# q, k and v laid out by chunk in DRAM, and no transposes of q and k, in a kernel of chunked attention and two mixtures of experts

## The chip, the cores and the metric

The kernel runs on one core of one Trainium2 chip. The core has five engines that run their own instruction streams and meet only through semaphores: TensorE (PE in the profile; its loads of the stationary operand are shown apart as PEld), VectorE (DVE), ScalarE (ACT), GpSimd (POOL) and SyncE (SP), which in this kernel only issues DMAs. Sixteen DMA engines move data between DRAM and the on-chip memory SBUF. The metric is the time of one execution on the device, in microseconds (us); lower is better.

## What is computed

Three stages follow each other. With 4 batches, 8 heads, 576 positions and 64 values per head there are 2304 tokens of 512 values.

```python
# attention inside chunks of 64 positions
q_c = q.reshape(B, H, nc, chunk, D)           # 4, 8, 9, 64, 64; k_c and v_c alike
scores = scale * np.matmul(q_c, k_c.transpose(0, 1, 2, 4, 3))
scores = scores - np.max(scores, axis=-1, keepdims=True)
attn = np.exp(scores)
attn = attn / (np.sum(attn, axis=-1, keepdims=True) + 1e-09)
out = np.matmul(attn, v_c)
x = np.ascontiguousarray(out.transpose(0, 2, 1, 3)).reshape(B * S, H * D)
# first mixture: all 4 experts, weighted
for e in range(4):
    h = np.maximum(x @ w1[e], 0.0)
    out += p[:, e:e + 1] * (h @ w2[e])
# second mixture: each token goes to the one of 8 experts with the largest logit
expert_idx = np.argmax(x @ w_gate, axis=1)
out[mask] = gate_w[mask, None] * (np.maximum(x[mask] @ w1[e], 0.0) @ w2[e])
```

All of it is float32. The inner size of the experts is 1024.

## The kernel before, in words

A tile is 128 tokens, that is two chunks of 64 positions with all 8 heads; there are 18 tiles, worked on in 6 groups of 3 (`TG`). Expert products are done with each operand split into a high and a low part, so a product is three matmuls; they are the lines 1214 to 1216 (first layer, `hidden`, 384 tokens wide) and 1245 to 1247 (second layer, `output`, 512 wide).

Attention of one tile has these stages. Its q and k come to `qin` and `kin` with tokens and heads on the partitions. PE transposes them (four transposes each, lines 1122 and 1127) into two PSUM banks; ACT copies q to `qT` in a block form whose other half is zero (`take_qT`, line 532), DVE copies k to `kT` (`take_kT`, line 709). PE multiplies them, one matmul for each head (`score`, line 1135). DVE subtracts the row maximum (`shift`, lines 715 and 716), ACT takes the exponential (line 537), DVE divides by the sum (`normalise`, lines 721 to 724). PE transposes the result (`transpose_p`, line 1143), ACT copies it (line 541), PE multiplies it with `vbd`, which holds v in block form (`attend`, line 1152), and ACT copies the result to `x` (line 549).

The attention of group 0 stands ahead of everything else ("the start" below). Its q and k arrive in staging tiles, `qst` and `kst`, and ACT and DVE first reorder them into `qin` and `kin` (lines 581 and 747). PE fills its pauses with matmuls on a tile of ones (`warm`, line 1182). Then come six groups for expert 0 of the first mixture; between their matmuls the attention of the *next* group is spread, by the table `STAGES`: a group has 16 steps (8 of `hidden`, 8 of `output`), and after a step PE, ACT and DVE each do the stages that the table names for it. So five groups (tiles 3 to 17) carry attention in this way. After them experts 1 to 3 and the second mixture run, which the change does not touch.

SP issues nearly all loads in one fixed order: the first q tiles, the first weight chunk, v of group 0 between further weight chunks, the small inputs, the rest of the 8 chunks of expert 0 (512 KB each), then q and k of tile 3 and of those behind. ACT issues the first k tiles. POOL rounds and splits each weight chunk of expert 0 (lines 442 and 436), and PE waits for chunk c before step 2c of the first group.

Of the kernel before, what the change touches and what calls it, by code (L numbers as in the profile page):

```python
# [5 lines left out]
def chunked_attention_then_two_moes(nc, q, k, v, domain_probs, w1, w2, w_gate, v1, v2, out):  # L6
# [10 lines left out]
    ds = bass.ds  # L17

    P = 128
    B, H, S, DH = q.shape  # L20
# [4 lines left out]
    C = 64  # L25
    NCH = S // C
    J = 4
    PJ = C // J
# [57 lines left out]
    qin = tile("qin", [P, TG, J, 2, DH], F32, a0)  # L86
    kin = tile("kin", [P, TG, J, 2, DH], F32, a0 + 6144)
    vbd = tile("vbd", [P, 2, KT, P], F32, a0 + 12288)
    qT = tile("qT", [P, H, P], F32, a0 + 16384)
    kT = tile("kT", [P, H, C], F32, a0 + 20480)  # L90
# [9 lines left out]
    qT0 = tile("qT0", [P, TG, H, P], F32, at["acc"] + 24576)  # L100
    kT0 = tile("kT0", [P, TG, H, C], F32, at["h"])
    qst = tile("qst", [P, TG, 2, J, DH], F32, at["h"] + 6144)
    kst = tile("kst", [P, TG, 2, J, DH], F32, at["h"] + 12288)
    assert at["acc"] + 36864 <= at["h"]
# [62 lines left out]
    def spare(name, shape, dtype):  # L167
# [3 lines left out]
        for n in shape[1:]:  # L171
# [24 lines left out]
    STAGES = {0: [("qk", 0)], 1: [("score", 0)], 4: [("p", 0), ("qk", 1)], 5: [("v", 0), ("score", 1)],  # L196
              8: [("p", 1), ("qk", 2)], 9: [("v", 1), ("score", 2)], 12: [("p", 2)], 13: [("v", 2)]}
# [9 lines left out]
    q_first = [sem(f"q_first{i}") for i in range(TG)]  # L207
    k_first = [sem(f"k_first{i}") for i in range(TG)]
# [44 lines left out]
    def chunk_of(src, g):  # L253

        a = src.rearrange("b h (n p j) d -> b n h p j d", n=NCH, j=J)
        return a[ds(g // NCH, 1), ds(g % NCH, 1)].rearrange("o u h p j d -> (o u h) p j d")

# [3 lines left out]
    with stack:  # L261
# [4 lines left out]
        def _(sp):  # L266
            def load_qk(t, j):

                for c in range(2):
                    for src, dst in ((q, qin), (k, kin)):  # L270
                        sp.dma_start(dst[:, j, :, c, :], chunk_of(src, t * 2 + c)).then_inc(qk_in[j], 16)

            def load_v(t, to=vbd[:, :, :, :], signal=v_in):

                for c in range(2):
                    g = t * 2 + c
                    for odd in range(2):
                        a = v.rearrange("b (r o) (n s) d -> b n o s r d", o=2, n=NCH)
                        a = a[ds(g // NCH, 1), ds(g % NCH, 1), odd].rearrange("o u s r d -> (o u s) r d")
                        sp.dma_start(to[odd * C:(odd + 1) * C, c, :, odd * DH:(odd + 1) * DH], a).then_inc(signal, 16)  # L280
# [33 lines left out]
            sp.wait_ge(sem("k_psum"), TG)  # L314
            load_qk(TG, 0)
            load_qk(TG + 1, 1)
            sp.wait_ge(sem("v_zeroed"), 1)
            load_v(TG)
            load_qk(TG + 2, 2)
# [84 lines left out]
        def _(pool):  # L404
# [6 lines left out]
            gp.memset(qT0[:, :, :, :], 0.0).then_inc(sem("q_zeroed"), 1)  # L411
            gp.memset(qT[:, :, :], 0.0).then_inc(sem("q_zeroed"), 1)
# [1083 lines left out]
```

## Time and profile before

| | |
|---|---|
| median of 3 runs | 1252.15 us (1249.66 to 1252.37) |
| the profiled execution, its own time | 1250.36 us |
| its span, from the first to the last instruction | 1248.6 us |
| PE busy | 1220.7 us of the span |
| TensorE clock granted, mean | 0.991 of full |
| DMA packets, bytes | 104449, 81.14 MB |
| packets under 512 B | 60831 |

Around the span lie 1250.36 - 1248.6 = 1.8 us that no instruction covers. A row of the timeline gives the start of a piece of work, how long it lasted and, in brackets, how long its engine had been idle and what ended that. Ends of matmuls are modelled, so the spacing of their starts tells what they cost.

### The profile page before, as it was taken

The numbers are of one execution on the slowest core, as the hardware profiler recorded it, in microseconds if no ns is written. First come the engines' busy times: TensorE is split into PE (matmuls) and PEld (weight loads), VectorE is DVE, ScalarE is ACT, GpSimd is POOL, SyncE is SP. The second block draws the span as 40 slices with busy tenths as digits, with TensorE's granted clock in tenths as the row PEclk, the third lists the DMA queues.
The fourth block names the chain that finished last, engine by engine and source line by source line (L and its number), as shares of the span: only waits on it lengthen the run. The fifth ranks groups of instructions, "written<-read, shape, count | busy, mean of one in ns | idle before, by whom it ended". The sixth has DMA issues, their size and how long they took to land.

```text
span 1248.6 us, 19074 instructions
## 1 busy us (share of the span) xinstructions
PE 1220.7 (98%) x6541; PEld 1082.1 (87%) x6542; DVE 475.4 (38%) x958; ACT 288.9 (23%) x455; POOL 316.9 (25%) x192
## 2 busy tenths in 40 slices
PE   8999999999999999999999999999997999999986
PEld 6999989989999999999999998899985888888875
DVE  5433434432222222222222223343355555555543
ACT  3322322323111113211111311222133011041420
POOL 7400000005000002300000601100047843085892
PEclk9999999999999999999999999999998999999998
DMA  7422122004000002100001300000174432272730
GB/s 203 117 51 50 37 59 51 21 9 135 1 0 0 0 0 84 50 0 0 0 0 35 100 26 27 0 25 25 63 189 121 122 122 94 65 241 79 245 131 21
DMA packets 104449, 81.14 MB, mean 65 GB/s; under 512 B 60831, under 2 KB 87071, under 8 KB 104418
## 3 DMA queue, kind: packets, MB, share of 16 engines
q1 hardware_dynamic: 99186, 68.67, 18.8%
q0 software_dynamic: 4416, 11.30, 2.8%
q10 hardware_dynamic: 816, 0.79, 0.2%
q8 instruction: 16, 0.26, 0.1%
q14 instruction: 15, 0.12, 0.0%
HBM read 71.12 MB, written 10.92 MB: 66 GB/s over the span
## 4 chain that ended last, share of the span: by engine, by line
PE 90%; SPq 3%; POOL 2%; DMA 1%; issue 1%; DVE 1%; ACT 1%; POOLq 0%; ACTq 0%; DVEq 0%
PE psum L1214 14%; PE psum L1216 14%; PE psum L1215 13%; PE psum L1245 10%; PE psum L1247 10%; PE psum L1246 10%; PE psum L1417 3%; PE psum L1419 3%; PE psum L1418 3%; PE psum L1135 2%; PE psum L1152 2%; POOL weights_r L436 2%; PE psum L1404 1%; PE psum L1264 1%; SPq L280 1%
## 5 line engine op out<-in xcount | busy, mean ns | idle before, releaser
L436 POOL TENSOR_TENSOR weights_r<-weights,weights_r 128x1024 fp32r<-128x1024 f32 x96 | 232.1, 2445 | 693.4 <-ACT weights_r L611 692.4
L1214 PE MATMUL psum<-xhi,weights_r 128*128 128x384 f32 x768 | 261.5, 340 | 1.1 <-DVEq L784 0.4
L1216 PE MATMUL psum<-xhi,weights_r 128*128 128x384 f32 x768 | 257.1, 335 | 0.0
L1215 PE MATMUL psum<-xlo,weights_r 128*128 128x384 f32 x768 | 256.9, 334 | 0.0
L1245 PE MATMUL psum<-weights_r,hhi 128*128 128x512 f32 x576 | 228.7, 397 | 0.0
L1247 PE MATMUL psum<-weights_r,hlo 128*128 128x512 f32 x576 | 225.1, 391 | 0.0
L1246 PE MATMUL psum<-weights_r,hhi 128*128 128x512 f32 x576 | 224.6, 390 | 0.0
L606 ACT ACTIVATE hhi<-psum 128x384 fp32r<-128x384 f32 x192 | 94.5, 492 | 507.9 <-PE psum L1216 507.4
L790 DVE SCALAR_TENSOR_TENSOR hlo<-psum,hhi 128x384 fp32r<-128x384 f32 x192 | 107.0, 557 | 264.1 <-ACT hhi L606 264.1
L611 ACT ACTIVATE weights_r<-weights 128x1024 fp32r<-128x1024 f32 x88 | 92.3, 1058 | 241.4 <-DMA weights<-in_moe_w 241.4
L1214 PEld LDWEIGHTS psum<-xhi,weights_r 128*128 128x128 f32 x768 | 144.3, 188 | 4.3 <-DVE xlo L738 2.1
L1215 PEld LDWEIGHTS psum<-xlo,weights_r 128*128 128x128 f32 x768 | 144.3, 188 | 0.7
L1216 PEld LDWEIGHTS psum<-xhi,weights_r 128*128 128x128 f32 x768 | 144.1, 188 | 0.0
L1247 PEld LDWEIGHTS psum<-weights_r,hlo 128*128 128x128 f32 x576 | 108.1, 188 | 23.3
L1246 PEld LDWEIGHTS psum<-weights_r,hhi 128*128 128x128 f32 x576 | 108.3, 188 | 20.8
L1245 PEld LDWEIGHTS psum<-weights_r,hhi 128*128 128x128 f32 x576 | 108.2, 188 | 20.4
L1417 PE MATMUL psum<-weights_r,hThi 128*128 (+1 forms) x184 | 74.8, 406 | 2.3 <-DVE hTlo L1039 2.3
L809 DVE SCALAR_TENSOR_TENSOR acc<-psum,dp,acc 128x512 f32 x36 | 25.2, 751 | 134.5 <-PE psum L1247 134.5
L1214 PE MATMUL psum<-weights_r,xThi 128*128 x176 | 71.0, 403 | 4.2 <-POOL weights_r L436 4.0
L1418 PE MATMUL psum<-weights_r,hThi 128*128 (+1 forms) x184 | 73.0, 397 | 0.0
L1419 PE MATMUL psum<-weights_r,hTlo 128*128 (+1 forms) x184 | 72.9, 396 | 0.0
L1216 PE MATMUL psum<-weights_r,xTlo 128*128 x176 | 69.0, 392 | 0.0
(178 smaller groups left out, 1216.3 us busy)
## 6 DMA issues: line engine op xcount, KB each, us to landing
weights<-in_moe_w SPq DMA_DIRECT2D x96, 512.0 KB, 5.6
vbd<-in_v SPq DMA_DIRECT2D x72, 64.0 KB, 2.4
x_rows<-xfin SPq DMA_DIRECT2D x18, 256.0 KB, 2.1
qin<-in_q SPq DMA_DIRECT2D x30, 128.0 KB
kin<-in_k SPq DMA_DIRECT2D x30, 128.0 KB
kst<-in_k ACTq DMA_DIRECT2D x6, 128.0 KB
qst<-in_q SPq DMA_DIRECT2D x6, 128.0 KB
meta<-slot_table SPq DMA_DIRECT2D x25, 1.0 KB, 3.1
```

The costliest lines, as they stand in the source:

```text
L436: gp.tensor_tensor(rounded(set_, 1, c), raw(set_, c), rounded(set_, 0, c).bitcast(F32), ALU.subtract).then_inc(sem("w_lo"), 1)
L606: sc.activation(hhi_r[:, f, :], psum[:, H_B[f], 0:G], ACT.Relu).then_inc(sem("hhi_ready"), 1)
L790: vec.scalar_tensor_tensor(hlo_r[:, f, :], psum[:, H_B[f], 0:G], 0.0, hhi[:, f, :], ALU.max, ALU.subtract).then_inc(sem("hlo_ready"), 1)
L1214: mm(out_, ahi, bhi, start=(i == 0), stop=False)
L1215: mm(out_, ahi, blo, start=False, stop=False)
L1216: last = mm(out_, alo, bhi, start=False, stop=(i == n - 1))
L1245: mm(o_, hhi_r[:, f, toks], mat2(W_r, 0, 0, f), start=(f == 0), stop=False)
L1246: mm(o_, hhi_r[:, f, toks], mat2(W_r, 1, 0, f), start=False, stop=False)
L1247: last = mm(o_, hlo_r[:, f, toks], mat2(W_r, 0, 0, f), start=False, stop=(f == FT - 1))
L1417: mm(psum[:, Y2_B, :], hThi_r[:, f, :], mat2(W_r, 0, off, f), start=(f == 0), stop=False)
L1418: mm(psum[:, Y2_B, :], hThi_r[:, f, :], mat2(W_r, 1, off, f), start=False, stop=False)
L1419: last = mm(psum[:, Y2_B, :], hTlo_r[:, f, :], mat2(W_r, 0, off, f), start=False, stop=(f == FT - 1))
```

## The change

The host arranges q, k and v in DRAM before the launch, and the kernel reads them as they lie there:

- q and k lie by chunk as [64 values of a head, 8 heads, 64 positions]. So they arrive with the values of a head on the partitions, and PE's transposes of q and k, the reordering of the first tiles, and the copies `take_qT` and `take_kT` are gone. `qT` is written by two DMAs for each tile, each into one quarter of the block form, in pieces of 64 float32 (256 bytes); `kT` by one DMA, with 2048 contiguous bytes for each partition. Before, q and k came in four DMAs for each tile.
- `qT` and `kT` have three buffers, one for each tile of a group, and group 0 uses the same ones.
- v lies as [tile, odd or even head, position, chunk, head pair, value]; its load is two DMAs for each tile and not four, still in pieces of 256 bytes. For group 0, ACT issues them behind k, where SP issued them before.
- Only the halves that no DMA writes are zeroed, by POOL and DVE.
- The stage "qk" leaves `STAGES`. SP's loads of q and k for tile t + 2 wait for the scores of tile t - 1 (`s_psum`) in the place of its transposes (`k_psum`).

```diff
-    qin = tile("qin", [P, TG, J, 2, DH], F32, a0)
-    kin = tile("kin", [P, TG, J, 2, DH], F32, a0 + 6144)
-    qT = tile("qT", [P, H, P], F32, a0 + 16384)
-    kT = tile("kT", [P, H, C], F32, a0 + 20480)
+    qT = tile("qT", [P, TG, H, P], F32, a0)
+    kT = tile("kT", [P, TG, H, C], F32, a0 + 12288)
...
-    STAGES = {0: [("qk", 0)], 1: [("score", 0)], 4: [("p", 0), ("qk", 1)], 5: [("v", 0), ("score", 1)],
-              8: [("p", 1), ("qk", 2)], 9: [("v", 1), ("score", 2)], 12: [("p", 2)], 13: [("v", 2)]}
+    STAGES = {1: [("score", 0)], 4: [("p", 0)], 5: [("v", 0), ("score", 1)],
+              8: [("p", 1)], 9: [("v", 1), ("score", 2)], 12: [("p", 2)], 13: [("v", 2)]}
...
+    q_rows = q.rearrange("b n d h s -> (b n d) h s")
+    k_rows = k.rearrange("b n d h s -> (b n d) h s")
...
                 for c in range(2):
-                    for src, dst in ((q, qin), (k, kin)):
-                        sp.dma_start(dst[:, j, :, c, :], chunk_of(src, t * 2 + c)).then_inc(qk_in[j], 16)
+                    sp.dma_start(qT[c * DH:(c + 1) * DH, j, :, c * C:(c + 1) * C],
+                                 q_rows[ds(t * P + c * DH, DH)]).then_inc(qk_in[j], 16)
+                sp.dma_start(kT[:, j, :, :], k_rows[ds(t * P, P)]).then_inc(qk_in[j], 16)
...
-                    sp.wait_ge(sem("k_psum"), t)
+                    sp.wait_ge(sem("s_psum"), t)
                     load_qk(t + 2, (j + 2) % TG)
...
-                    sp.dma_start(qst[:, j, c, :, :], chunk_of(q, j * 2 + c)).then_inc(q_first[j], 16)
-            load_w(0, w1, w2, 0, 0)
-            sp.wait_ge(sem("v0_zeroed"), 1)
-            load_v(0, vbd0[:, 0:2, :, :], v_first[0])
-            load_w(0, w1, w2, 0, 1)
-            load_v(1, vbd0[:, 2:4, :, :], v_first[1])
-            load_v(2, vbd0[:, 4:6, :, :], v_first[2])
-            load_w(0, w1, w2, 0, 2)
+                    sp.dma_start(qT[c * DH:(c + 1) * DH, j, :, c * C:(c + 1) * C],
+                                 q_rows[j * P + c * DH:j * P + (c + 1) * DH]).then_inc(qk_in[j], 16)
+            for c in range(TG):
+                load_w(0, w1, w2, 0, c)
...
             for j in range(TG):
-                for c in range(2):
-                    act.dma_start(kst[:, j, c, :, :], chunk_of(k, j * 2 + c)).then_inc(k_first[j], 16)
+                act.dma_start(kT[:, j, :, :], k_rows[j * P:(j + 1) * P]).then_inc(qk_in[j], 16)
                 if j == 0:
                     act.wait_ge(sem("ones_ready"), 1)
                     sc.activation(lshift[:, :], ones[:, 0:E2], ACT.Exp)
...
+            for j in range(TG):
+                for odd in range(2):
+                    act.dma_start(vbd0[odd * C:(odd + 1) * C, 2 * j:2 * j + 2, :, odd * DH:(odd + 1) * DH], v[j, odd])\
+                        .then_inc(v_first[j], 16)
...
-                    if stage == "qk":
+                    if stage == "score":
+                        pe.wait_ge(qk_in[j], (g + 1) * 48)
                         pe.wait_ge(sem("shifted"), t)
-                        pe.wait_ge(qk_in[j], g * 64)
-                        transpose_q(t, j, Q_B)
-                        pe.wait_ge(sem("x_ready"), t - (j > 0))
-                        transpose_k(t, j, K_B)
-                    elif stage == "score":
-                        score(t)
+                        score(t, j)
...
+            pe.wait_ge(sem("q_zeroed"), 2)
+            for j in range(TG):
+                pe.wait_ge(qk_in[j], 48)
+                score(j, j, Q0_B[j], warm)
             pe.wait_ge(sem("ident_ready"), 1)
-            for j in range(TG):
-                pe.wait_ge(sem("q_ordered"), j + 1)
-                transpose_q(j, j, Q0_B[j])
-                pe.wait_ge(sem("k_ordered"), j + 1)
-                transpose_k(j, j, K0_B[j])
-                warm(3)
-                if j:
-                    score(j - 1, Q0_B[j - 1], qT0[:, j - 1, :, :], kT0[:, j - 1, :, :], warm)
-            score(TG - 1, Q0_B[TG - 1], qT0[:, TG - 1, :, :], kT0[:, TG - 1, :, :], warm)
+            pe.wait_ge(sem("v0_zeroed"), 2)
             warm(6)
...
```

The order of the instructions changes at three places that the text below speaks of. First PE, from its first instruction on, before the change; `qT_73` and `kT_74` are the tiles of group 0, and what an instruction waits for stands in brackets:

```order
L1182 MATMUL psum<-ones 128x512 x8
L1122 MATMUL psum<-ident,qin 128x128 [waits q_ordered,ident_ready]
L1122 MATMUL psum<-ident,qin 128x128 x3
L1127 MATMUL psum<-ident,kin 128x128 [waits k_ordered]
L1127 MATMUL psum<-ident,kin 128x128 x3
L1182 MATMUL psum<-ones 128x512 x3
L1122 MATMUL psum<-ident,qin 128x128 [waits q_ordered]
L1122 MATMUL psum<-ident,qin 128x128 x3
L1127 MATMUL psum<-ident,kin 128x128 [waits k_ordered]
L1127 MATMUL psum<-ident,kin 128x128 x3
L1182 MATMUL psum<-ones 128x512 x3
L1135 MATMUL psum<-kT_74,qT_73 128x64 [waits kT_ready,qT_ready]
```

The same place on PE after the change, where line 1106 is `warm` and line 1063 is `score`:

```order
L1106 MATMUL psum<-ones 128x512 x8
L1063 MATMUL psum<-kT,qT 128x64 [waits qk_in0,q_zeroed]
L1063 MATMUL psum<-kT,qT 128x64 x2
L1106 MATMUL psum<-ones 128x512
L1063 MATMUL psum<-kT,qT 128x64 x3
L1106 MATMUL psum<-ones 128x512
L1063 MATMUL psum<-kT,qT 128x64 x2
L1063 MATMUL psum<-kT,qT 128x64 [waits qk_in1]
```

The scores now follow the loads directly: the waits on `q_ordered`, `k_ordered`, `qT_ready` and `kT_ready` are replaced by one wait for each tile's DMAs.

Second, PE in the loop over the groups, behind step 0 (the last matmul of it stands first), before the change:

```order
L1216 MATMUL psum<-xhi,weights_r 128x384
L1163 REGISTER_ALU
L1164 REGISTER_ALU [waits shifted]
L1122 MATMUL psum<-ident,qin 128x128 [waits qk_in0]
L1122 MATMUL psum<-ident,qin 128x128 x3
L1127 MATMUL psum<-ident,kin 128x128 [waits x_ready]
L1127 MATMUL psum<-ident,kin 128x128 x3
L1214 MATMUL psum<-xhi,weights_r 128x384
```

After the change nothing stands behind step 0, and behind step 1 (lines 1135 to 1137 are now the products of the first layer) there is:

```order
L1137 MATMUL psum<-xhi,weights_r 128x384
L1091 ISA
L1092 REGISTER_ALU [waits qk_in0]
L1063 MATMUL psum<-kT,qT 128x64 [waits shifted]
L1063 MATMUL psum<-kT,qT 128x64 x7
L1147 ISA [waits w_lo]
```

Eight transposes for each tile have left PE's stream, and the wait for q and k of a group's first tile has moved from behind step 0 to behind step 1. Third, SP from its first DMA on, before the change:

```order
L295 DMA qst<-in_q 128x1x256 x6
L283 DMA weights_50<-in_moe_w 128x4x256
L280 DMA vbd_70<-in_v 64x4x64 [waits v0_zeroed]
L280 DMA vbd_70<-in_v 64x4x64 x3
L283 DMA weights_50<-in_moe_w 128x4x256
L280 DMA vbd_70<-in_v 64x4x64 x8
L283 DMA weights_50<-in_moe_w 128x4x256
```

And after the change, down to q and k of tile 3:

```order
L280 DMA qT<-in_q 64x8x64 x6
L268 DMA weights_50<-in_moe_w 128x4x256 x3
L284 DMA dp<-in_moe_domain_probs 128x18x4
L285 DMA wg<-in_moe_w_gate 128x4x8
L268 DMA weights_50<-in_moe_w 128x4x256
L268 DMA weights_51<-in_moe_w 128x2x512
L290 DMA slot_table<-fill 128x302 [waits filled]
L292 DMA x_rows<-zrow 1x512
L268 DMA weights_51<-in_moe_w 128x2x512 x3
L257 DMA qT<-in_q 64x8x64 [waits s_psum]
L257 DMA qT<-in_q 64x8x64
L259 DMA kT<-in_k 128x512
```

The twelve DMAs of v have left SP's order; ACT issues six in their place, ahead of its first exponential.

## Rows read from the trace of the kernel before

**Rows 1.** The page: busy time by engine, and the chain by engine.

```profile
PE 1220.7 (98%) x6541; PEld 1082.1 (87%) x6542; DVE 475.4 (38%) x958; ACT 288.9 (23%) x455; POOL 316.9 (25%) x192
...
PE 90%; SPq 3%; POOL 2%; DMA 1%; issue 1%; DVE 1%; ACT 1%; POOLq 0%; ACTq 0%; DVEq 0%
```

**Rows 2.** Busy time in one stretch: stretch, length, engines, clock, DMA share, GB/s.

```profile
83.00:126.00 43.00, 43.00 (x278) 40.57 (x277) 17.31 (x32) 12.04 (x22) 0.00 (x0) 1.00 0.22 50
```

**Rows 3.** Groups of PE from 32 to 258 us: line, shapes, count | busy, mean ns.

```profile
L1122 PE MATMUL psum<-ident,qin 128*128 128x128 f32 x60 | 9.0, 273 | 0.9 <-DMA kin<-in_k 0.9
L1127 PE MATMUL psum<-ident,kin 128*128 128x128 f32 x60 | 9.0, 273 | 0.0
```

**Rows 4.** Timeline of PE from 60 to 90 us: start, duration, line.

```profile
60.88 0.60 PE L1143 MATMUL psum<-ident,probs 128*128 128x128 f32 x4
61.31 0.60 PE L1122 MATMUL psum<-ident,qin 128*128 128x128 f32 x4
...
62.42 0.40 PE L1246 MATMUL psum<-weights_r,hhi 128*128 128x512 f32 x1
...
74.02 0.60 PE L1143 MATMUL psum<-ident,probs 128*128 128x128 f32 x4
...
74.69 0.39 PE L1246 MATMUL psum<-weights_r,hhi 128*128 128x512 f32 x1
...
84.73 0.34 PE L1216 MATMUL psum<-xhi,weights_r 128*128 128x384 f32 x1
84.90 0.60 PE L1122 MATMUL psum<-ident,qin 128*128 128x128 f32 x4
...
85.95 0.34 PE L1215 MATMUL psum<-xlo,weights_r 128*128 128x384 f32 x1
```

**Rows 5.** Timeline of the start: zeroing, and the waits for k of tiles 0, 1, 2.

```profile
1.53 2.65 POOL L411 MEMSET qT<- 128x3072 f32 x1
...
6.77 1.00 DVE L747 COPY kin<-kst 128x512 f32<-128x512 f32 x1 [2.59 <-DMA kst<-in_k]
...
9.99 0.43 DVE L747 COPY kin<-kst 128x512 f32<-128x512 f32 x1 [2.22 <-DMA kst<-in_k]
...
13.52 0.43 DVE L747 COPY kin<-kst 128x512 f32<-128x512 f32 x1 [2.50 <-DMA kst<-in_k]
```

**Rows 6.** Timeline of the start: PE from the second score on.

```profile
15.98 0.78 PE L1135 MATMUL psum<-kT,qT 128*128 128x64 f32 x6
...
20.14 1.46 PE L1182 MATMUL psum<-ones 128*128 128x512 bf16 x6
...
21.56 0.66 PE L1143 MATMUL psum<-ident,probs 128*128 128x128 f32 x4
...
33.29 0.44 PE L1214 MATMUL psum<-xhi,weights_r 128*128 128x384 f32 x1 [0.39 <-DVEq L784]
```

**Rows 7.** Timeline of the start: issues of SP.

```profile
5.89 3.38 SPq L280 DMA_DIRECT2D vbd<-in_v  x4
...
10.15 7.67 SPq L280 DMA_DIRECT2D vbd<-in_v  x8
...
32.83 1.00 SPq L271 DMA_DIRECT2D kin<-in_k  x1
```

**Rows 8.** Four stretches, with the columns of rows 2.

```profile
8.00:10.00 2.00, 1.94 (x10) 1.03 (x10) 0.01 (x1) 1.19 (x3) 0.66 (x4) 0.68 0.97 288
10.00:12.00 2.00, 2.00 (x9) 1.34 (x8) 1.02 (x2) 0.51 (x1) 0.00 (x0) 0.50 0.92 223
18.00:20.00 2.00, 2.00 (x19) 1.95 (x19) 1.66 (x3) 0.24 (x1) 1.92 (x2) 1.00 0.30 64
36.00:38.00 2.00, 1.41 (x11) 1.41 (x12) 0.84 (x2) 0.90 (x3) 2.00 (x2) 1.00 0.62 141
```

**Rows 9.** Timeline: POOL's first weight chunk, and PE at tile 3.

```profile
14.50 1.04 POOL L442 CAST weights_r<-weights 128x1024 fp32r<-128x1024 f32 x1 [5.78 <-DMA weights<-in_moe_w]
...
36.59 0.66 PE L1122 MATMUL psum<-ident,qin 128*128 128x128 f32 x4 [0.93 <-DMA kin<-in_k]
```

More of the change, by code:

```diff
@@ L99, in chunked_attention_then_two_moes @@
     pT0 = tile("pT0", [P, TG, KT, P], F32, at["acc"] + 18432)
[L100 to L104, printed above, removed]
+    assert at["acc"] + 24576 <= at["h"]
     rows = tile("rows", [P, NB, D], F32, at["acc"])
@@ L522, in _ @@
             sc = nc.scalar
-            def take_qT(t, bank=Q_B, to=qT[:, :, :]):
-                act.wait_ge(sem("q_psum"), t + 1)
-                for c in range(2):
-                    lanes = slice(c * C, (c + 1) * C)
-                    src = psum[lanes, bank, :].rearrange("x (j h p) -> x h p j", j=J, h=H)
-                    dst = to[lanes, :, c * C:(c + 1) * C].rearrange("x h (p j) -> x h p j", j=J)
-                    last = sc.activation(dst, src, ACT.Copy)
-                last.then_inc(sem("qT_ready"), 1)
             def exponentials(t, p=probs[:, :, :]):
@@ L576, in _ @@
                     sc.activation(lshift[:, :], ones[:, 0:E2], ACT.Exp)
-            def order_q(j):
-                act.wait_ge(q_first[j], 32)
-                sc.activation(qin[:, j, :, :, :], qst[:, j, :, :, :].rearrange("x c m d -> x m c d"), ACT.Copy)\
-                    .then_inc(sem("q_ordered"), 1)
-            order_q(0)
-            order_q(1)
-            act.wait_ge(sem("q_zeroed"), 1)
-            take_qT(0, Q0_B[0], qT0[:, 0, :, :])
-            order_q(2)
-            for j in range(1, TG):
-                take_qT(j, Q0_B[j], qT0[:, j, :, :])
+            for j in range(TG):
+                for odd in range(2):
+                    act.dma_start(vbd0[odd * C:(odd + 1) * C, 2 * j:2 * j + 2, :, odd * DH:(odd + 1) * DH], v[j, odd])\
+                        .then_inc(v_first[j], 16)
             for j in range(TG):
@@ L1117, in _, with score @@
             mm, tr = nc.tensor.matmul, nc.tensor.transpose
-            def transpose_q(t, j, bank):
-                for m in range(J):
-                    last = tr(psum[:, bank, m * P:(m + 1) * P], qin[:, j, m, :, :].rearrange("p c d -> p (c d)"), ident[:, :])
-                last.then_inc(sem("q_psum"), 1)
-            def transpose_k(t, j, bank):
-                for m in range(J):
-                    last = tr(psum[:, bank, m * P:(m + 1) * P], kin[:, j, m, :, :].rearrange("p c d -> p (c d)"), ident[:, :])
-                last.then_inc(sem("k_psum"), 1)
-            def score(t, bank=Q_B, q_=qT[:, :, :], k_=kT[:, :, :], between=None):
-                pe.wait_ge(sem("qT_ready"), t + 1)
-                pe.wait_ge(sem("kT_ready"), t + 1)
+            def score(t, j, bank=Q_B, between=None):
                 for h in range(H):
-                    last = mm(psum[:, bank, h * C:(h + 1) * C], q_[:, h, :], k_[:, h, :], start=True, stop=True)
+                    last = mm(psum[:, bank, h * C:(h + 1) * C], qT[:, j, h, :], kT[:, j, h, :], start=True, stop=True)
                     if between is not None and h in (2, 5):
@@ L1476, with _laid_out @@
 _INS = ["q", "k", "v", "moe_domain_probs", "moe_w1", "moe_w2", "moe2_w_gate", "moe2_w1", "moe2_w2"]
+_CHUNK = 64
+def _laid_out(name, a):
+    import numpy as np
+    if name in ("q", "k"):
+        b, h, s, d = a.shape
+        a = a.reshape(b, h, s // _CHUNK, _CHUNK, d).transpose(0, 2, 4, 1, 3)
+    if name == "v":
+        b, h, s, d = a.shape
+        a = a.reshape(b, h // 2, 2, s // _CHUNK, _CHUNK, d).transpose(0, 3, 2, 4, 1, 5)
+        a = a.reshape(-1, 2, 2, _CHUNK, h // 2, d).transpose(0, 2, 3, 1, 4, 5)
+    return np.ascontiguousarray(a)
 def kernel(**inputs):
-    import numpy as np
     import concourse.bacc as bacc
```

70 lines of the change are left out of this document (21 added, 49 removed).

## The prediction

> **What bounds the kernel now.** I read the page first: PE is busy for 1220.7 of 1248.6 us and makes up 90% of the chain that ended last, while no other engine is above 38% [rows 1]. Then the stretches: in a group that carries attention PE is busy 43.00 of 43.00 us at full clock, with the DMA engines at 0.22 of their time [rows 2]. So in the five groups with attention whatever leaves PE's stream shortens the program, and ACT's and DVE's copies and the loads lie beside it. The other place is the start, before 33.29 us, where PE does its first real expert product [rows 6]. There the timeline shows PE waiting for q and k: the k of tiles 0, 1 and 2 lands at 6.77, 9.99 and 13.52 us [rows 5], and what PE fills in between are matmuls on ones. A third place is tile 3, whose k makes PE wait 0.93 us at 36.59 [rows 9].
>
> **The transposes in the loop.** The groups of PE from 32 us on show 60 transposes of q and 60 of k, that is 4 + 4 for each of 15 tiles [rows 3]. Their mean is 273 ns, but they overlap: four transposes take from 60.88 to 61.31, 0.43 us [rows 4]. What a tile's eight cost, with the change of form at their edges, I take from equal places with and without them. From a first transpose of the probabilities to the second matmul of the next product it is 62.42 - 60.88 = 1.54 us where those of q and k stand between, and 74.69 - 74.02 = 0.67 us where they don't: 0.87 us. At a group's first tile, where they stand alone, it is 85.95 - 84.73 = 1.22 us, less two normal steps of 84.90 - 84.73 = 0.17: 0.88 us [rows 4]. 15 x 0.875 = 13.1 us go. Nothing takes their place: between a tile's score and its transposed probabilities the same three steps stand as before, and the copies of q and k that left ACT and DVE can only bring those chains forward. The bounds are 11 us (120 x 0.43 / 4 = 12.9 for the transposes alone, less some 2 should the wait for q and k now cost PE something at each tile) and 13.5.
>
> The Trainium skill, "TensorE: Matmul & The Clock Gate", Part 4 (PE-mode transpose), gives about 275 ns for a transpose inside a kernel and says that PE's access to SBUF makes up most of it. The mean in the groups agrees (273 ns), the spacing of the starts does not (0.11 us). By the page the loop would give back 120 x 0.275 = 33 us.
>
> **The start.** Removed there are the reordering, 24 transposes, the copies, and 9 filling matmuls. Scores now follow the landing of q and k. What stands behind the last landing, L, is: one score with its two fillers, of which two take from 15.98 to 20.14, so 2.1 us; six fillers, 1.5 us; and then the unchanged run from the first transposed probabilities at 21.56 to the product at 33.29, 11.7 us [rows 6]. The product starts at L + 15.3. DVE's softmax is not later than that: its first tile's scores are there by some 9 us, and the six fillers stand where it once was the last. The zeroing of the blocks, 2.65 us from 1.53 on for the whole of it [rows 5] and about half as much now, is over before the first landing; the zeroing of v's blocks, two more such pieces, before v is used.
>
> When is L? Of 1.57 MB for three tiles, k comes in 3 DMAs in place of 6 and in longer pieces; q comes in 256-byte pieces, a quarter of the 1 KB ones before. At 8 to 10 us, when mostly 1 KB pieces moved, the engines gave 288 GB/s at a share of 0.97; at 36 to 38, with 256-byte pieces, 141 GB/s at 0.62, which would be 227 at a full share [rows 8]. So q costs a quarter more engine time and k less. The nearest rows are the landings themselves, 3.2 and 3.5 us apart, and I keep L = 13.5 [rows 5]. Bounds: the last 0.52 MB at 288 GB/s behind the landing at 9.99 gives L = 11.8; the last two tiles at half of 141 GB/s, the other half going to v and weights on the other queues, 1.05 MB in 14.9 us behind 6.77, gives L = 21.7. With L = 13.5 the product starts at 28.8, a gain of 4.5 us; the bounds give 6.2 us gained and 3.7 us lost.
>
> The Trainium skill, "DMA: Bandwidth & Descriptors", Specifications, asks for at least 512 bytes for a transfer at line rate, and that speaks against q's new pieces. The rows agree in direction, 227 against 297 GB/s at a full share. Were it half the rate, q's 0.79 MB would need 5.3 us in place of 2.6, and L would be at most 2.7 us later.
>
> TensorE's clock was 0.68 of full at 8 to 10 us and 0.50, the lower level of 1.2 GHz, at 10 to 12, behind its pause before the first transposes, and full at 18 [rows 8]. PE will again pause between landings, and with less filling. If the low level lasts into the last score, that is 2 us more; it belongs to the bound above.
>
> v of group 0 is issued by ACT, behind k and ahead of its first exponential. The 12 DMAs of v cost SP 3.38 + 7.67 us [rows 7]; six of twice the size may hold ACT until some 11 us, about when the first scores are shifted, and v is first used at L + 5. I cost it at nothing; if ACT is held 5 us longer, half of that shows. The first weight chunk landed at 14.50 [rows 9], with v in front of part of it; POOL's 3.4 us for each chunk end long before 28.8, and behind it PE needs a chunk every 4.3 us.
>
> **Tile 3.** Its k landed at 36.54, from an issue that began at 32.83 [rows 7, 9]. It is now needed behind two steps, at 28.8 + 4.3 = 33.1. SP no longer spends 11 us on v before it, but the bytes ahead of it are the same, and the engines are near full from 20 us on. What I count is the slack that issuing v left: at 18 to 20 the share was 0.30 [rows 8], 1.4 us. That gives 35.1, a stall of 2.0 us; with all of SP's time as gain there is no stall. I take 0.9, between them, which cancels the 0.93 that goes; the bounds are +0.9 and -1.1 us.
>
> **The sum.** 13.1 + 4.5 + 0.0 = 17.6 us off the profiled execution's 1250.36: 1232.8. That execution is 1.8 us below the median of 1252.15; in terms of the median it is 1234.5, and I say 1234.3. Later stages only move forward as a whole. The forecast's own range is 1231 to 1238.
>
> **The rivals.**
>
> *The start gives nothing* (0.20). The smaller pieces, the low clock or ACT held by its issues delay the last score by some 4.5 us, or the start's gain turns into a longer wait for tile 3. For it: the engines are near full at 8 to 12 us [rows 8], and the same bytes must come. Against: PE's chain behind L is shorter by its copies whatever L is. 1250.4 - 13.1 = 1237.3, median 1239.
>
> *Early landing* (0.12). k and q come as fast as at 8 to 10 us and tile 3 is in time: 13.1 + 6.2 + 0.9 = 20.2, so 1230.2, median 1232.
>
> *The loop is not shorter* (0.03). Another chain takes the room of the transposes. Against it: PE is without a pause in rows 2. Only 4.5 us are gained: 1245.9, median 1247.7.
>
> *Each transpose counts in full* (0.01). 120 x 0.273 = 32.8 us, as the means of rows 3 would have it; with the start 1213, median 1215. Four in 0.43 us exclude nearly all of it.
>
> *Slower* (0.04). One mechanism: the start starves on small pieces. At 18 to 20 us the core took only 64 GB/s, when v's 256-byte pieces were issued [rows 7, 8]. If everything before the first product (q, k, v of group 0 and one weight chunk, 2.88 MB) moved at that rate it would be there at 45 us behind the first landings' 2 us, the product at 47, and tile 3's 0.52 MB 8 us later: 21.8 lost against 13.1 gained, 1259, median 1261. It decides once the product starts later than 33.29 + 13.1 = 46.4 us. Against it, other stretches of such pieces show 141 GB/s, and the 64 is a queue that one issuer held back.
>
> The chances are 0.60 for the forecast, then 0.20, 0.12, 0.03, 0.01 and 0.04. The range of 1228 to 1241 takes in both neighbours of the forecast and the bound of L. About 0.2% (2.5 us) is what a measurement can tell from no change. Every case but the last lies beyond it on the fast side, with a hundredth for one that falls short: faster 0.95, the same 0.01, slower 0.04.
>
> **What would show it.** In the changed profile, PE from 32 us on without the 120 transposes, and the five groups with attention together 13 us shorter; the first product near 28.8 us; the wait for q or k of tile 3 near 0.9 us; no wait of PE for `qT` or `kT` in later groups. A first product later than 31 us, waits of PE at tiles 4 to 17, or a low clock beyond 14 us would make the forecast wrong.

## The result, and the profile after

The changed kernel took 1232.6 us (median of 4 runs, 1226.76 to 1234.42) beside 1250.91 us for the kernel before (4 runs, 1249.29 to 1252.37): ratio 0.985, 95% interval 0.9829 to 0.9871, so 18.3 us between the medians, 1.5% faster. The forecast was 1234.3 us. In e0_again below it was 0.9853 (0.9838 to 0.9868). Ratios leave out runs in a slower state of the chip; among those reported here that is one of the ten of e7_before_fill18, 1520.95 us at a mean granted clock of 0.75.

The profiled execution took 1234.42 us, with a span of 1232.6 us. The page shows, at the places of [rows 1]:

```profile
PE 1207.6 (98%) x6388; PEld 1070.5 (87%) x6389; DVE 462.6 (38%) x939; ACT 267.2 (22%) x416; POOL 315.5 (26%) x192
...
DMA packets 92639, 81.11 MB, mean 66 GB/s; under 512 B 48255, under 2 KB 72959, under 8 KB 92610
```

PE is as full as before, with 153 instructions fewer in the record: 144 transposes and 9 fillers. What its time is made of shows best at the places where a group starts. The kernel before, timeline of PE at the starts of its second and third group:

```profile
82.71 0.44 PE L1214 MATMUL psum<-xhi,weights_r 128*128 128x384 f32 x1
...
130.99 0.44 PE L1214 MATMUL psum<-xhi,weights_r 128*128 128x384 f32 x1
...
888.94 0.33 PE L1214 MATMUL psum<-xhi,weights_r 128*128 128x384 f32 x1
```

The changed kernel at the same places, with the first group's start ahead of them; the last row of each is the start of the last group of the first mixture:

```profile
34.24 0.45 PE L1135 MATMUL psum<-xhi,weights_r 128*128 128x384 f32 x1 [0.39 <-DVEq L724]
...
79.85 0.44 PE L1135 MATMUL psum<-xhi,weights_r 128*128 128x384 f32 x1
...
125.48 0.44 PE L1135 MATMUL psum<-xhi,weights_r 128*128 128x384 f32 x1
...
875.54 0.33 PE L1135 MATMUL psum<-xhi,weights_r 128*128 128x384 f32 x1
```

A group with attention takes 125.48 - 79.85 = 45.63 us in place of 48.28. By stretches the 16.0 us between the two spans are:

| stretch | before | after | gained |
|---|---|---|---|
| the start, to the first expert product | 33.29 | 34.24 | -0.95 |
| first group with attention | 49.42 | 45.61 | 3.81 |
| the four groups behind it | 193.16 | 182.61 | 10.55 |
| on to the last group of the first mixture | 613.07 | 613.08 | -0.01 |
| from there to the end | 359.66 | 357.06 | 2.60 |

The last stretch scatters by 3 us from profile to profile (355.55 to 358.60 us with the new layout), so its 2.60 is of one pair only. So the groups gave what was expected, and the start gave nothing. The start of the changed kernel, timeline of PE (start, duration, line, and the idle time before it):

```profile
1.26 4.02 PE L1106 MATMUL psum<-ones 128*128 128x512 bf16 x9 [1.26 <-POOL ones L388]
7.35 1.51 PE L1063 MATMUL psum<-kT,qT 128*128 128x64 f32 x6 [2.08 <-DMA qT<-in_q]
8.66 0.63 PE L1106 MATMUL psum<-ones 128*128 128x512 bf16 x1
9.08 1.38 PE L1063 MATMUL psum<-kT,qT 128*128 128x64 f32 x6
...
19.54 2.77 PE L1106 MATMUL psum<-ones 128*128 128x512 bf16 x6
22.10 1.06 PE L1071 MATMUL psum<-ident,probs 128*128 128x128 f32 x4
```

Three heads of a score, the six records at 9.08, take 1.38 us; in [rows 6] the same six took 0.78. The six fillers take 2.77 in place of 1.46.
```profile
1.25 4.02 PE L1182 MATMUL psum<-ones 128*128 128x512 bf16 x9 [1.25 <-POOL ones L407]
6.54 0.63 PE L1122 MATMUL psum<-ident,qin 128*128 128x128 f32 x4 [1.27 <-ACT qin L581]
...
10.48 1.11 PE L1127 MATMUL psum<-ident,kin 128*128 128x128 f32 x4
```

### The profile page after: what moved, and what is told of

Read it like the earlier page. It is cut to its first block, busy times and chain, and to the rows that moved or that the text cites. A ratio compares the mean times of both kernels' runs of the same rounds, so it can differ in the third digit from the quotient of the medians.

```text
span 1232.6 us, 18555 instructions
## 1 busy us (share of the span) xinstructions
PE 1207.6 (98%) x6388; PEld 1070.5 (87%) x6389; DVE 462.6 (38%) x939; ACT 267.2 (22%) x416; POOL 315.5 (26%) x192
## 4 chain that ended last, share of the span: by engine, by line
PE 91%; issue 2%; POOL 2%; DMA 2%; DVE 1%; ACT 1%; POOLq 0%; SPq 0%; DVEq 0%; ACTq 0%
PE psum L1135 14%; PE psum L1137 14%; PE psum L1136 14%; PE psum L1166 10%; PE psum L1168 10%; PE psum L1167 10%; PE psum L1338 3%; PE psum L1063 3%; PE psum L1340 3%; PE psum L1339 3%; PE psum L1080 3%; POOL weights_r L417 2%; PE psum L1325 1%; PE psum L1185 1%; DMA weights<-in_moe_w 1%
```

## The experiments

Each kernel is the changed kernel with the edit shown, unless said otherwise. The first product (its start, us) and the first group with attention (its length, us) are from one profile each, as above.

| run | median us (runs) | ratio to before, interval | first product | first group |
|---|---|---|---|---|
| e0_again | 1232.34 (4) | 0.9853, 0.9838 to 0.9868 | 34.10 | 45.61 |
| e1_fill18 | 1229.65 (5) | 0.9836, 0.9822 to 0.9849 | 28.55 | 46.36 |
| e2_tr_loop | 1246.33 (6) | 0.9966, 0.9954 to 0.9978 | 33.79 | 48.23 |
| e3_dense | 1232.54 (4) | 0.9851, 0.9836 to 0.9866 | 33.02 | 45.63 |
| e4_v_on_sp | 1230.12 (4) | 0.9832, 0.9809 to 0.9854 | 27.41 | 47.03 |
| e5_q_long_pieces | 1293.76 (4) | 1.0345, 1.0324 to 1.0366 | 33.30 | 58.07 |
| e6_fill12 | 1232.53 (4) | 0.9864, 0.9842 to 0.9886 | 27.32 | 46.88 |
| e7_before_fill18 | 1249.85 (10) | 1.0001, 0.9990 to 1.0012 | 32.44 | 49.44 |
| e9_tile3_early | 1227.61 (5) | 0.9828, 0.9811 to 0.9845 | 27.73 | 46.11 |
| e10_both | 1226.70 (5) | 0.9815, 0.9801 to 0.9829 | 26.51 | 46.59 |
| e11_fill12_again | 1232.18 (4) | 0.9855, 0.9839 to 0.9872 | 33.89 | 45.60 |
| e12_before_again | 1248.46 (11) | 1.0000, 0.9991 to 1.0009 | 33.16 | 49.53 |

**e0_again: nothing edited.** 

> The changed kernel once more, with nothing edited, for the spread of its executions and a second profile. In the first profile TensorE ran at its low level from the first score (7.35 us) until about 22 us, and the first expert product started at 34.24 us. Theory A (the clock of the start decides: the scores with one filler each three heads leave TensorE too idle for the high level, and whether and when it rises differs from one execution to the next): times scatter over 1226 to 1235 us, and in a faster execution the first product starts earlier by what it is faster. Rival B (the scatter comes from the tail, from waits behind gathered rows): the first product stands at 34.2 us whatever the time.

The first product stood at 34.10 us, as in the first profile, and the last stretch was 355.9 us in place of 357.1. The times scatter by 3 us here. So part of the scatter is the tail's, as rival B had it; whether a fast start is the other part was not tested, since this profile caught none.

**e2_tr_loop: the transposes' time put back.**

```diff
+                if step in (0, 4, 8):
+                    t = g * TG + step // 4
+                    pe.wait_ge(sem("shifted"), t)
+                    for r in range(4):
+                        tr(psum[:, Q_B, r * P:(r + 1) * P], ident[:, :], ident[:, :])
+                    pe.wait_ge(sem("x_ready"), t - (step > 0))
+                    for r in range(4):
+                        tr(psum[:, K_B, r * P:(r + 1) * P], ident[:, :], ident[:, :])
```

The identity stands in for q and k; nobody reads the results.

> The changed kernel with the eight transposes of each tile put back into TensorE's stream in the five groups with attention, at the old steps and into the same banks, reading the identity tile in place of q and k (nobody uses their results); the copies of ScalarE and VectorE, the loads and the start stay as changed. Theory A (the loop's gain is TensorE's time for the transposes, 0.88 us for each tile): each of the five groups is 2.64 us longer, 48.3 us again, and the time rises by 13.2 us against the changed kernel. Rival (part of the gain came from the copies or the lighter loads): less than 11 us comes back.

It took 14.0 us more than e0_again. Its timeline at the starts of the second and third group:

```profile
82.02 0.44 PE L1143 MATMUL psum<-xhi,weights_r 128*128 128x384 f32 x1
...
130.30 0.44 PE L1143 MATMUL psum<-xhi,weights_r 128*128 128x384 f32 x1
```

130.30 - 82.02 = 48.28 us, to the hundredth that of the kernel before. The four later groups are 2.6 us longer each (0.88 for each tile), the first 2.62. The rival falls: the copies of ACT and DVE and the lighter loads gave nothing in the loop; it was PE's time alone.

Its start is that of the changed kernel, and its clock record begins early enough to show it. Windows (stretch, length, engines, granted clock, DMA share, GB/s):

```profile
7.00:9.00 2.00, 1.11 (x7) 1.15 (x8) 0.00 (x0) 0.00 (x0) 0.38 (x2) 0.85 1.38 198
9.00:11.00 2.00, 2.00 (x10) 1.82 (x10) 0.00 (x0) 0.00 (x0) 0.00 (x0) 0.50 1.35 209
```

Here the clock was high for a moment and fell within the first score, behind a pause of 2.69 us; it was still at 0.50 from 20 to 22 us. So three profiles with this start, of after, e0_again and e2_tr_loop, have the low level through the scores, by two ways: it never rose, or it fell after the pause.

**e1_fill18 and e3_dense: what holds the clock down.** The first has twice the fillers, and so a shorter pause behind them (1.10 us in place of 2.08):

```diff
-            warm(9)
+            warm(18)
```

> 18 fillers in place of 9 ahead of the first score, so that TensorE has no pause before q and k of tile 0 land at 7.35 us. Theory A1 (the 2.08 us pause is what keeps the clock low): the clock rises during the fillers and stays high, scores take 2.1 us each in place of 4, the first product comes at 25 to 29 us, and the time falls by 5 to 9 us against the changed kernel, to about 1225 us. Theory A2 (the mix of scores and few fillers is too thin for the high level, with or without the pause): the clock is high for the first score at most and falls again; the first product at 32 to 34 us, time within 2 us of the changed kernel. Rival C (landing of q and k bounds the start, not the clock): the first product stays at 34 us and the scores wait for DMAs.

```profile
1.26 6.02 PE L1106 MATMUL psum<-ones 128*128 128x512 bf16 x18 [1.26 <-POOL ones L388]
8.37 0.85 PE L1063 MATMUL psum<-kT,qT 128*128 128x64 f32 x6 [1.10 <-DMA qT<-in_q]
...
13.41 0.88 PE L1063 MATMUL psum<-kT,qT 128*128 128x64 f32 x6 [0.47 <-DMA qT<-in_q]
...
28.55 0.45 PE L1135 MATMUL psum<-xhi,weights_r 128*128 128x384 f32 x1 [0.39 <-DVEq L724]
...
33.26 1.99 PE L1063 MATMUL psum<-kT,qT 128*128 128x64 f32 x16 [0.25 <-DMA kT<-in_k]
```

18 fillers end in 6 us, which is less than twice what 9 took, so the level rises within them. It stays up through the scores with the same thin mix: three heads in 0.85 us in place of 1.51. The scores now do follow the landings, the last at 13.41 us, and the first product comes at 28.55 us, 5.6 us earlier. So the landings were not what held the start at 34 us (rival C), and the thin mix did not bring the level down (theory A2). Whether the shorter pause did it, as theory A1 says, or the greater number of fillers, this run can't tell, since it changes both. The median fell by 2.7 us and not 5 to 9, and the two sets of times overlap (1227.88 to 1231.85 against 1230.39 to 1233.42): the first group is 0.75 us longer, some of it a wait for k of tile 3 that was hidden before, and the last stretch of this profile is 1.45 us longer than that of e0_again.

The second leaves the pause and adds fillers inside the scores:

```diff
-                score(j, j, Q0_B[j], warm)
+                score(j, j, Q0_B[j], lambda n: warm(3 * n))
```

> Three fillers in place of one at each of the two places inside a score of the start (12 more fillers of 512 columns in all, 2.6 us at full clock, 5.1 us at half). Theory A2 (thin mix keeps the clock low): the denser mix raises the clock by about 12 us; the first product at 30 to 33 us, time 1 to 4 us less than the changed kernel. Theory A1 (the pause alone decides): the clock stays low as before and the product comes 3 to 5 us later, 1236 to 1240 us.

```profile
12.20 1.49 PE L1106 MATMUL psum<-ones 128*128 128x512 bf16 x3
...
14.78 0.81 PE L1106 MATMUL psum<-ones 128*128 128x512 bf16 x3
```

The level rose at about 14 us and the first product came at 33.02 us, 1.1 us earlier than in e0_again, though q of tile 0 had landed 1.2 us later; theory A2 had said 30 to 33. The median did not move: the fillers cost most of what the clock gave, and the last stretch of this profile is the longest of all (358.60 us). Taken together, in these runs the thin mix kept a high level and did not bring a low one up, and a denser one did.

**e6_fill12 and e11_fill12_again: one kernel, two starts.** `warm(9)` becomes `warm(12)`.

> 12 fillers in place of 9 (e1_fill18 had 18); at the low level they end at 6.4 us, at the high level near 6.1, so the pause before the first score is 1 to 2 us. If three more fillers are enough for the clock to be high when the first score starts, its six matmuls take about 0.85 us as in e1_fill18 and the first product stands near 28.5 us; if not, they take 1.5 us and the product stands at 34 us, as with 9.

> The kernel with 12 fillers once more, for its two kinds of execution: its four times were 1227.09 (the profiled one, high clock at the start, first product at 27.32 us), 1231.2, 1233.86 and 1234.87. Theory (the clock of the start is high in some executions and low in others, which is worth the 7 us between first products at 27.3 and 34.2 us, less 1.3 us of waiting for tile 3): times again spread over 6 to 8 us, wider than those of e1_fill18 (1227.88 to 1231.85), and a profile that falls on a slow execution shows scores of some 4 us. Rival (the spread comes from the tail alone, which differed by up to 3 us between profiles): all times within 4 us.

The two profiles fell on different starts. That of e6_fill12:

```profile
1.25 5.05 PE L1106 MATMUL psum<-ones 128*128 128x512 bf16 x12 [1.25 <-POOL ones L388]
7.07 0.85 PE L1063 MATMUL psum<-kT,qT 128*128 128x64 f32 x6 [0.76 <-DMA qT<-in_q]
```

That of e11_fill12_again, and its windows:

```profile
1.25 4.25 PE L1106 MATMUL psum<-ones 128*128 128x512 bf16 x12 [1.25 <-POOL ones L388]
8.27 1.51 PE L1063 MATMUL psum<-kT,qT 128*128 128x64 f32 x6 [2.77 <-DMA qT<-in_q]
```

```profile
6.00:8.00 2.00, 0.00 (x0) 0.00 (x0) 0.00 (x0) 0.00 (x0) 1.37 (x7) 0.92 1.36 196
8.00:10.00 2.00, 1.73 (x7) 1.68 (x8) 0.00 (x0) 0.00 (x0) 0.00 (x0) 0.50 1.38 201
...
18.00:20.00 2.00, 2.00 (x10) 1.82 (x10) 1.82 (x5) 0.63 (x1) 2.00 (x2) 0.50 0.59 41
```

Here q of tile 0 landed 1.2 us later, the pause was 2.77 us and not 0.76, and the granted clock, which had risen within the fillers (12 in 4.25 us), fell in the pause and stayed at 0.50 beyond 20 us. The first product stood at 27.32 us in the one execution and at 33.89 in the other. These are two profiles, but they carry the theory that one kernel has both starts. The expected wide scatter did not come back: the four times of the second run lie within 2.5 us (1230.47 to 1232.97), those of the first within 7.8 (1227.09, the profiled one, to 1234.87).

**e7_before_fill18: the two starts with the same fillers.** The kernel before with `warm(18)`.

> The kernel before, with 18 fillers in place of 9 ahead of its first transposes. It compares the two starts with the same fillers. In the kernel before TensorE's clock was at its low level only from about 8.7 to 12 us. If fillers keep it high there, the first product comes up to 1.5 us earlier than 33.29 us, near 32; if the start is bound by the landing of q and k (13.52 us for k of tile 2), it stays within 0.5 us of 33.3. Against e1_fill18's 28.55 the changed start would then be worth 3.5 to 4.8 us, near the 4.5 us of the forecast.

The first product came at 32.44 us, 0.85 earlier, and the median did not move (1.0001). Here the clock stayed high (three fillers at 8.32 took 0.81 us, where they took 1.10 in the kernel before). Against e1_fill18 the changed start is worth 32.44 - 28.55 = 3.9 us when both have a high clock, one profile against one.

**e4_v_on_sp and e5_q_long_pieces: what sets the landings.** Both keep the 18 fillers. In the first SP issues v of group 0 behind the first weight chunk:

```diff
             for c in range(TG):
                 load_w(0, w1, w2, 0, c)
+                if c == 0:
+                    for j in range(TG):
+                        for odd in range(2):
+                            sp.dma_start(vbd0[...], v[j, odd]).then_inc(v_first[j], 16)
...
             for j in range(TG):
-                for odd in range(2):
-                    act.dma_start(vbd0[...], v[j, odd]).then_inc(v_first[j], 16)
```

> 18 fillers as in e1_fill18, and the six loads of v of group 0 issued by SyncE behind the first weight chunk in place of ScalarE. In e1_fill18 TensorE waits for q of tile 0 until 8.37 us and for q of tile 2 until 13.41 us, and the first product stands at 28.55 us. Theory C1 (v and weights on the other queue share the DMA engines with q and make it late): q of tile 0 lands at 6 to 7 us and q of tile 2 at 11 to 12, the first product comes 1 to 2 us earlier. Rival C2 (q's own 256-byte pieces, or how fast they are issued, set the landings): both waits stay within 0.5 us. Either way the loads of tile 3 may come later, since SyncE issues v ahead of them; if that costs more than the start gains, the time is that of e1_fill18 or above.

PE met no wait for q or k of the three tiles (the last score began at about 11.7 us, so tile 2 had landed at least 1.7 us earlier than the 13.41 of e1_fill18). The six loads of q show it directly; the time from issue to landing, shortest, median and longest, in e1_fill18 and in e4_v_on_sp:

```profile
DMA to landing us min/median/max: 3.0/7.1/9.0
```

```profile
DMA to landing us min/median/max: 4.4/5.1/5.2
```

The longest is 5.2 us here and 5.3 in e10_both, which has v on SP too, and 7.9 to 9.8 in the eight profiles with v on ACT and q in short pieces. So C1 holds: v beside q delays q. The Trainium skill, "DMA: Bandwidth & Descriptors", Issuing engines are not separate DMA queues, says that DMAs issued by SP and by ACT run on the same sixteen engines; these landings agree: loads that ACT issued lengthened those of SP.

What that is worth is less clear. The first product came 1.1 us earlier than in e1_fill18, but e6_fill12, with v on ACT, has it at 27.32 us, as early as here. And it was given back at tile 3, where PE waited 1.05 us for k; both kernels reach the second group within 0.5 us of each other (74.44 and 74.91), and the medians do not differ:

```profile
32.92 1.99 PE L1064 MATMUL psum<-kT,qT 128*128 128x64 f32 x16 [1.05 <-DMA kT<-in_k]
```

The second stores q with the heads innermost, and reads the stationary operand with a stride:

```diff
-    qT = tile("qT", [P, TG, H, P], F32, a0)
+    qT = tile("qT", [P, TG, P, H], F32, a0)
...
-                    last = mm(psum[:, bank, h * C:(h + 1) * C], qT[:, j, h, :], kT[:, j, h, :], start=True, stop=True)
+                    last = mm(psum[:, bank, h * C:(h + 1) * C], qT[:, j, :, h], kT[:, j, h, :], start=True, stop=True)
```

> 18 fillers as in e1_fill18, and q laid out with the heads innermost, so that q's DMAs write pieces of 2 KB in place of 256 bytes; in exchange the stationary operand of the scores is read with a stride of 8 elements. Rival C2 of the run with v on SyncE (the pieces' size sets the landings): q of tile 0 lands by 7 us, tile 2 by 12, the first product at 26 to 27.5 us. Theory C1: landings within 0.5 us of e1_fill18. If the strided read of the stationary operand costs TensorE time, each score is longer than 2.1 us, and the five groups with attention grow beyond 45.6 us.

It took 44 us more than the kernel before and 64 more than e1_fill18, for another reason than the one asked about. The groups of PE's loads of the stationary operand, line | busy, mean ns, here and in e1_fill18:

```profile
L1063 PEld LDWEIGHTS psum<-kT,qT 128*128 128x128 f32 x288 | 70.5, 334 | 0.8 <-issue 0.5
```

```profile
L1063 PEld LDWEIGHTS psum<-kT,qT 128*128 128x128 f32 x288 | 34.6, 192 | 3.0 <-issue 2.1 <-DMA qT<-in_q 0.6
```

A stationary operand read with a stride of 32 bytes takes 334 ns to load and not 192. Each group with attention grew by 12.4 us, and that is not the loads alone. The last score of the second group and the product behind it, and that group's window with its granted clock, here and in e1_fill18:

```profile
128.14 4.01 PE L1063 MATMUL psum<-kT,qT 128*128 128x64 f32 x16
131.91 0.77 PE L1166 MATMUL psum<-weights_r,hhi 128*128 128x512 f32 x1
...
91.37:149.39 58.02, 57.90 (x277) 53.73 (x277) 17.60 (x31) 10.85 (x18) 0.00 (x0) 0.85 0.15 41
```

```profile
103.81 1.95 PE L1063 MATMUL psum<-kT,qT 128*128 128x64 f32 x16
105.57 0.48 PE L1166 MATMUL psum<-weights_r,hhi 128*128 128x512 f32 x1
...
74.91:120.54 45.63, 45.51 (x276) 42.03 (x276) 17.42 (x31) 10.85 (x18) 0.00 (x0) 1.00 0.20 52
```

The first of the three scores, 95.67 to 99.33 us, ran at a granted clock of 1.00 and took 3.66 us all the same, so the longer load is not the clock's doing. A score takes 3.77 us in place of 1.76, so three take some 6.0 us more. The other half of the 12.4 us lies in the work behind them: during or after each score the granted clock fell to 0.50, though PE had no pause, and expert products 384 wide stood 0.32 us apart in place of 0.17. The first score began at 6.76 us without a wait, and the clock fell at about 11.4 us, so PE shows no later landing. The loads themselves do: from issue to landing the six of q took 5.6 us in the median and at most 8.1, in the eight profiles with short pieces and v on ACT 6.0 to 7.2 and at most 7.9 to 9.8. So pieces of 2 KB did not bring the last landing forward beyond the scatter, against rival C2.

**e9_tile3_early and e10_both: the order of the loads.** Both keep the 18 fillers. The loads of tile 3 take the place of the small `wg`, which moves behind those of tile 5:

```diff
-            sp.dma_start(wg[:, :, :], w_gate.rearrange("(t p) e -> p t e", p=P)).then_inc(sem("wg_in"), 16)
+            sp.wait_ge(sem("s_psum"), 1)
+            load_qk(TG, 0)
...
             sp.wait_ge(sem("s_psum"), 2)
-            load_qk(TG, 0)
...
             load_qk(TG + 2, 2)
+            sp.dma_start(wg[:, :, :], w_gate.rearrange("(t p) e -> p t e", p=P)).then_inc(sem("wg_in"), 16)
```

> 18 fillers as in e1_fill18; SyncE issues q and k of tile 3 ahead of the weight chunks 3 to 7, in the place of the small gate matrix (wg), which goes behind the loads of tile 5 (it is first used some 900 us later). In the runs with a high clock at the start TensorE waited for k of tile 3 until 32.8 to 33.3 us, whether the first product came at 27.3 or 28.6 us. Theory (tile 3's place in the queue is the next bound of the start): no wait at tile 3, the first group with attention takes 45.6 us again in place of 46.4, the first product stays near 28.5 us, and the time falls by about 0.8 us against e1_fill18, to 1229. Rival: the weight chunks now come too late, and TensorE waits for POOL's split of a chunk in the first group, which is then longer than 46 us.

> The same as e9_tile3_early, and v of group 0 issued by SyncE behind the first weight chunk, as in e4_v_on_sp, where the first product came at 27.41 us. Theory: first product at 27.4 us and a first group of 45.6 us, 1.9 us less than e1_fill18, some 1228 us. Rival: v or a weight chunk is late: TensorE waits for v in the start or for a chunk in the first group.

What the place in SP's queue costs does not hang on the load that stands there: the issue of `wg`, 16 KB, held SP for 6.83 us from 11.27 us on in the changed kernel, and here that of the first load of q of tile 3 for 6.90 us from 11.23 us on. PE no longer waits for tile 3 in either. The first group of e9_tile3_early is 46.11 us, 0.25 less than that of e1_fill18 and not the 45.6 of the theory; PE has one short wait in it, 0.18 us for DVE. In e10_both, which adds the edit of e4, the first product comes at 26.51 us; the first group is still 1 us over its 45.6, and PE waits there 0.66 us for DVE:

```profile
39.65 0.66 PE L1073 MATMUL psum<-ident,probs 128*128 128x128 f32 x4 [0.66 <-DVE probs L681]
```

With 1226.7 us (1225.75 to 1227.18) e10_both is the fastest and the steadiest of all: 1.85% below the kernel before (0.9801 to 0.9829, clear of the 0.9838 to 0.9868 of e0_again), and 5.6 us below the changed kernel's 1232.34. The two medians were not taken side by side, and the kernel before measured beside each differs by 1.05 us.

**e12_before_again: the tail.** 

> The kernel before once more, with nothing edited, for a third profile of its tail. From the start of the last group of the first mixture to the end of the span, its two profiles so far (one of them with more fillers at the start) took 359.7 and 359.9 us, and eleven profiles of kernels with the new layout 355.6 to 358.6. Theory T (the tail is really some 2.8 us shorter with the new layout): above 359 us again. Rival (chance: the tail waits for gathered rows, whose landing scatters): 356 to 358.6 us.

The last stretch was 358.93 us. The three profiles of the old layout have 358.93, 359.66 and 359.92, the eleven of the new one 355.55 to 358.60, mean 356.9. They don't overlap, which speaks for theory T, though 358.93 lies just under the 359 that it asked for and only 0.33 us above the longest of the new ones.

## Why the prediction came out right, step by step

**The loop: right.** 13.1 us were forecast for 15 tiles at 0.875. The five groups lost 14.36 us, of which 0.93 is the wait for tile 3 of [rows 9], so 13.4 us. e2_tr_loop, which put only PE's transposes back, restored the four later groups to within 0.01 us. Reading the distance between equal places [rows 4] and not the mean duration [rows 3] was what made the number good.

**The start: wrong in mechanism.** The step that failed is "the product starts at L + 15.3" with the clock's part held to 2 us. The landings were judged well: 13.41 us for the last with a high clock, where 13.5 was said, and then the product at 28.55, where 28.8 was said. But in the kernel as it is that chain was not the bound. TensorE ran at 1.2 GHz from its first filler until about 23 us, a score took 4 us and not 2.1, and the product came at 34.24: 0.95 us lost in place of 4.5 gained. The kernel before had a high level at 6.5 us, and the low one that followed ended at about 12 us [rows 8]; the changed kernel has nine fillers fewer there, those behind the transposes, and e3_dense, which puts twelve into the scores, raised the level at 14 us. The Trainium skill, "TensorE: Matmul & The Clock Gate", Part 1, calls the lower level the default that activity releases. That agrees with the fillers' effect in e1_fill18 and e3_dense. It does not say by itself that PE can be without a pause from 7.35 to 23 us, as here, and stay at the low level. The rival "the start gives nothing" named the low clock, and in the profiled executions it is what happened. The runs with 18 and with 9 fillers show it: 28.55 against 34.10 us. With a high clock in both kernels the changed start was worth 3.9 us (e7_before_fill18), near the 4.5 forecast. Of the prediction's own signs of being wrong, two are there: a first product later than 31 us, and a low clock beyond 14 us.

**Tile 3: a cost that this kernel did not pay.** 0.9 us of waiting was forecast for a product at 28.8 us, to cancel the 0.93 that goes. With its product at 34.2 us PE finds tile 3's data there, so the 0.93 us of waiting went and nothing took its place. Where the clock was high, a wait appeared: 0.25 us in e1_fill18 with its product at 28.55, less than forecast (its first group is 0.75 us longer in all), and 1.05 in e4_v_on_sp with its product at 27.41, and the second group started at 74.2 to 74.9 us in three kernels whose first products were up to 1.2 us apart.

**v on ACT: half right.** It held up no exponential: the first came at 13.12 us, right behind DVE's subtraction. What I had not counted is that it shares the DMA engines with q from 2.3 us on: up to 9.8 us from issue to landing of q in place of 5.2.

**The rest: not forecast.** "Later stages only move forward as a whole" missed 2.6 us in the last stretch. So the sum on the profiled pair, 16.0 us against 17.6, is a loop that held (0.3 more), a start off by 5.4 us, 0.93 us more from tile 3, and a tail that made up for half of what the start lacked. That these cancel is chance. So may be part of the median: the changed kernel's start has, by all that e6 and e11 show for 12 fillers, a high clock in some executions, and its fastest run, 1226.76 us, is where such a start would put it; no profile of this start caught one that kept it, so that is argued and not shown.

What stays open is why the last stretch is shorter with the new layout. The transposes are not it, since e2_tr_loop has 356.86 us. A wait for gathered rows is in it: PE waited for `xs` 3.8, 5.4 and 2.9 us in the three old profiles and 1.5 to 3.8 in the new ones. What the layout of q, k and v has to do with it no run shows.

## What to carry to other kernels

What work costs on a full engine is the distance between equal places with and without it. Its recorded duration overlaps its neighbours'. Work that is removed from a start also removes activity: compare the spacing of equal matmuls there with that of a place at full clock, also where the granted clock reads 1.00 before its first change, and try more fillers before looking for faster loads. When a start gets shorter, the next load in the queue is its new bound, so reorder the queue with it.

## What was not expected of the hardware

- The same thin mix of fp32 scores and fillers ran for 15 us at the low level without rising (7.35 to 22 us), and at the high level without falling (e1_fill18). Behind a pause of 0.76 us the clock was high and within one of 2.77 us it fell, in two executions of one kernel.
- A stationary fp32 operand of 128 columns read with a stride of 8 elements loads in 334 ns in place of 192. A score of 8 matmuls then takes 3.77 us in place of 1.76, and the granted clock falls during or after it though PE has no pause (0.85 over a group in place of 1.00), so that a group with three scores is 12.4 us longer (58.02 against 45.63 us), about half of it by each.
- Loads issued by ACT beside those of SP lengthened q's landing from at most 5.3 to as much as 9.8 us; pieces of 2 KB in place of 256 bytes did not shorten it beyond the scatter (8.1 us).
